# Attention of a fused kernel: value matmuls per head in one burst instead of one block per query tile, scores one tile ahead, partial blocks made full

## The chip, the cores and the metric

One core of one Trainium2 chip runs the whole program. The metric is the device time in microseconds of one execution. All data is float32; some matmul operands are rounded to a float32 form that TensorE takes in one pass (`F32R`), the others are streamed in two passes.

## The reference

Three stages in a row: attention with a threshold, a mixture of experts with one expert per token, and a second MLP. Only the first is touched by the change.

```python
def _attn_ref(q, k, v, tau):                 # q, k, v: (4, 8, 576, 64)
    scale = 1.0 / np.sqrt(q.shape[-1])
    scores = scale * np.matmul(q, k.transpose(0, 1, 3, 2))
    thresh = np.max(scores, axis=-1, keepdims=True) - tau
    scores = np.where(scores >= thresh, scores, -1000000000.0)
    scores = scores - np.max(scores, axis=-1, keepdims=True)
    attn = np.exp(scores)
    attn = attn / (np.sum(attn, axis=-1, keepdims=True) + 1e-09)
    return np.matmul(attn, v)
...
    x = attn_out.transpose(0, 2, 1, 3).reshape(B * S, H * D)
    x = _moe_ref(x=x, ...)                   # softmax gate, argmax expert, relu MLP
    return _moe2_ref(x=x, ...)               # g = h * sigmoid(1.702 h), second matmul
```

## The kernel before

Attention runs over 32 heads (4 sequences by 8 heads), taken in pairs; `b` is 0 or 1 within a pair. The 576 query rows of a head make five tiles of 128 rows, of which the last has 64 (`TPB` = 5, `LAST` = 64). A tile is a unit `n` of 160. Each engine has its own program, a Python loop written out for ten units of a pair and repeated over the pairs (`over_pairs`), and engines wait for each other on semaphores. There is no scheduler: the order on an engine is that of the code. Each engine works on a unit at another delay.

- POOL (`split_step`, lines 521 to 530) splits q and k into a rounded part and the rest, `qk_parts`, for a head two later. It also computes `thresh` (L568) and copies `vv` (L577, L578).
- TensorE, step of unit `n`: scores of `n` (L1140, four passes of 288 columns into one of two buffers `s_ps`); then `transpose`, which turns the probabilities of unit `n - 3` (four blocks at L1103, then three blocks of `qk_parts` at L1118, then the fifth block of probabilities at L1103) into `pt_ps`, which has one buffer; then the value block `j` of a unit eight back (L1167): two matmuls, of 256 and 320 columns, with 64 columns of `vv` as weights, one into the lower and one into the upper half of the partitions of `o_ps`. Five such blocks add up to a head.
- ScalarE: `copy_turned` copies `pt_ps` out (L939, L942 into `pT`, L947 into `qkT`), then the exponential of unit `n` (L968). In tile 2 of a head it also copies `o_ps` of an earlier head to `oT` (L962, L963).
- DVE: scores out of `s_ps` with their maximum (L662), the bias for the exponential (L666), then the mask of unit `n - 2` (L646), which multiplies the probabilities and sums them. In tile 4 it also writes x and the gate shares of an earlier head from `misc` ("x parts", L679 and L683), in tile 2 the sums' inverse (L692, L695).
- The turn (L1150) on TensorE, in tile 4: `oT` with an identity and the gate weights, three blocks of 128, 128 and 64 rows into `misc`.

What the others wait for: the transposes of unit `n - 3` wait for its mask (`probs_ready`) and for ScalarE's copy of the last ones (`keys_copied`, `turned_copied`); scores of `n` wait for the maximum of `n - 2` (`max_ready`). The semaphore `pv_block` counts value blocks.

Of the kernel before, what the change touches and what calls it, by code (L numbers as in the profile page):

```python
# [16 lines left out]
P = 128  # L17


def attention_moe_mlp_kernel(nc, q, k, v, tau, modality_id, w_gate, modality_bias, w1, w2, w_in, w_out, out):  # L20
# [45 lines left out]
    with ctx:  # L66
# [42 lines left out]
        placed[0] = max(placed[0], routing_end)  # L109
        oT = put("oT", [P, UP])  # L110

# [145 lines left out]
        pv_ready = sem("pv_ready")  # L257
        pv_block = sem("pv_block")
        oT_copied = sem("oT_copied")
# [110 lines left out]
        def _(sp):  # L370
# [63 lines left out]

            sp.wait_ge(pv_block, UNITS)
            sp.wait_ge(y_filled, (SLOTS - NT - 1) * 16)
# [73 lines left out]
        def _(pool):  # L510
# [49 lines left out]
            def step(pair):  # L560
                for b in range(2):
                    for t in range(TPB):
# [9 lines left out]
                        if t == 4:  # L572
                            head = pair * 2 + b
                            wait(pool, v_loaded[b], (pair + 1) * V_LOADS)

                            wait_apart(pool, pv_block, (head - 1) * TPB)
                            pool.tensor_copy(vv[b][:, 0:TPB - 1], v_in[b][:, 0:TPB - 1]).then_inc(v_copied, 1)  # L577
                            pool.tensor_copy(vv[b][0:LAST, TPB - 1], v_in[b][0:LAST, TPB - 1]).then_inc(v_copied, 1)  # L578
# [37 lines left out]
        def _(dve):  # L616
            dve.memset(row_sum[:], 1.0).then_inc(tau_ready, 1)
            for b in range(2):
                dve.memset(qk[b][LAST:P, TPB - 1], 0.0).then_inc(pads_cleared, 1)
                dve.memset(vv[b][LAST:P, TPB - 1], 0.0).then_inc(pads_cleared, 1)  # L620
            dve.memset(oT[0:DH, LOW:UP], 0.0).then_inc(pads_cleared, 1)
# [28 lines left out]
            def step(pair):  # L650
                for b in range(2):
                    for t in range(TPB):
# [3 lines left out]
                        if on(n, 0, UNITS):  # L656
# [268 lines left out]
        def _(act):  # L925
# [3 lines left out]

            def copy_turned(m, u, b, t, with_probs, with_qk):  # L930

                ub, ut = u // TPB, u % TPB
                w = rows(ut)
                if with_probs:
                    if ut == 0:

                        wait(act, pv_block, m - BEHIND - TPB)
                    act.wait_ge(keys_turned, m - BEHIND + 1)
                    act.copy(pT[ub][:, 0:TPB - 1, ut * P:ut * P + w], pt_ps[:, 0:TPB - 1, 0:w]).then_inc(keys_copied, 1)  # L939
# [10 lines left out]
            def step(pair):  # L950
                for b in range(2):
                    for t in range(TPB):
# [3 lines left out]
                        if on(n, 0, UNITS + 3):  # L956
                            copy_turned(n + AHEAD, (b * TPB + t - 3) % (2 * TPB), (b * TPB + t + AHEAD) // TPB % 2, (t + AHEAD) % TPB,
                                        on(n, 3, UNITS + 3), on(n, 0, UNITS - AHEAD))
# [12 lines left out]
            for m in range(AHEAD):  # L971
                copy_turned(m, 0, m // TPB, m % TPB, False, True)
            act.wait_ge(tau_ready, 5)
# [120 lines left out]
        def _(pe):  # L1094
            pe.wait_ge(consts, 3)

            def transpose(m, u, b, t, with_probs, with_qk):
# [25 lines left out]
            for m in range(AHEAD):  # L1123
                transpose(m, 0, m // TPB, m % TPB, False, True)

            def step(pair):
                for b in range(2):
                    for t in range(TPB):
                        n = pair * (2 * TPB) + b * TPB + t
                        head = pair * 2 + b  # L1130
                        r = rows(t)
                        if on(n, 0, UNITS):
                            if t == 0:

                                wait(pe, turned_copied, n + TPB)

                            wait(pe, max_ready, n - 1)
                            for c in range(2):
                                for part in (1, 2):
                                    mm = pe.matmul(s_ps[(b * TPB + t) % 2][:, c, 0:HALF], qkT[b][:, 0, t * P:(t + 1) * P],  # L1140
                                                   qkT[b][:, part, c * HALF:(c + 1) * HALF],
                                                   start=(part == 1), stop=(part == 2))
                            mm.then_inc(scores_ready, 1)
                        if t == 4 and on(head, 2, NH + 2):
                            wait(pe, oT_copied, head - 1)
                            wait(pe, x_written, (head - 2) * 4)
                            of_head = bass.ds((pair - 1) % (HEADS // 2) * 2 + b, 1)
                            for i in range(3):
                                w = min(P, UP - i * P)
                                mm = pe.matmul(misc[0:w, i * 2 * XW:(i + 1) * 2 * XW], oT[:, i * P:i * P + w],  # L1150
                                               turn_and_gate[:, of_head].rearrange("p a h w -> p (a h w)"),
                                               start=True, stop=True)
                            mm.then_inc(o_written, 1)
                        if on(n, 0, UNITS + 3):
                            transpose(n + AHEAD, (b * TPB + t - 3) % (2 * TPB), (b * TPB + t + AHEAD) // TPB % 2, (t + AHEAD) % TPB,
                                      on(n, 3, UNITS + 3), on(n, 0, UNITS - AHEAD))
                        if on(n, 8, UNITS + 8):
                            u = (b * TPB + t - 8) % (2 * TPB)
                            ub, j = u // TPB, u % TPB
                            if j == 0:  # L1160

                                wait(pe, keys_copied, n - 8 + TPB)
                                wait(pe, turned_copied, n - 8 + BEHIND + TPB)
                                wait(pe, v_copied, head * 2)
                                wait(pe, oT_copied, head - 1)
                            for lo, at, w in ((0, 0, LOW), (DH, LOW, UP)):
                                mm = pe.matmul(o_ps[lo:lo + DH, 0:w], vv[ub][:, j, :], pT[ub][:, j, at:at + w],  # L1167
                                               start=(j == 0), stop=(j == TPB - 1))
                            mm.then_inc(pv_block, 1)

            pe.wait_ge(pads_cleared, 7)
            pe.wait_ge(gate_loaded, 2 * 16)
            over_pairs(pe, step, PAIRS + 1)


# [153 lines left out]
```

## Time and profile before

| What | Value |
|---|---|
| Median of 3 runs | 1176.48 us (1175.52 to 1178.59) |
| Profiled execution | its span is 1178.2 us; no other time of it is given |
| TensorE busy, whole span | 1078.6 us, 92% |
| TensorE, DVE, ScalarE busy, 24 to 439 us | 405.09, 343.97, 323.96 of 415 us |
| Granted TensorE clock, 24 to 439 us | 1.00 (2.4 GHz) |
| First scores matmul, last x part of attention | 19.09 us, 438.95 us |
| Share of `DVE row_sum_eps L692` in the chain that ended last | 2% |

The span is the time from the first to the last instruction of the profiled execution, here 1.7 us above the median. TensorE's matmuls overlap each other in the records, so one row of several passes lasts longer than the distance to the next row; distances between starts tell what a piece takes. Attention fills the first 439 us of the span. Its ten-unit body repeats without change, so one pair of heads tells the rest.

### The profile page before, as it was taken

The page shows a single profiled execution, that of the slowest core. Times are in us where ns is not written, and L with a number is a line of the kernel's source. Part 1 is how long each engine was busy: PE and PEld are TensorE (multiplying, and loading weights), DVE is VectorE, ACT ScalarE, POOL GpSimd, SP SyncE. Part 2 cuts the span into 40 slices and gives each one's busy share as a digit, 9 for nine tenths or more (in the row PEclk, how much of TensorE's full clock was granted, in tenths as well). Part 3 has the DMA queues.
Part 4 walks back from the last instruction along what each step waited for, and adds up shares of the span by engine and source line. Part 5 has one row for each costly group of instructions (what it writes and reads, how often), then busy time and mean ns, then how long its engine had stood idle before and what let it go on. Part 6 is the DMA issues. An engine that isn't in the chain of part 4 may idle for free.

```text
span 1178.2 us, 19745 instructions
## 1 busy us (share of the span) xinstructions
PE 1078.6 (92%) x6008; PEld 862.0 (73%) x6009; DVE 575.5 (49%) x1421; ACT 522.0 (44%) x1086; POOL 251.3 (21%) x433
## 2 busy tenths in 40 slices
PE   4999999999999982779999969499999999999998
PEld 3666666666666642658888847389899999999997
DVE  3888888888888865411222232265322322222221
ACT  3887778777878750412222232254222222222222
POOL 5554455455445300000010100201001010100000
PEclk9999999999999995889999989699999999999999
DMA  3142211211122012991111114222001000000000
GB/s 68 40 155 50 55 40 42 48 45 40 45 50 50 21 31 79 244 28 43 45 45 45 36 50 155 89 82 63 27 2 53 0 27 27 27 27 0 27 1 27
DMA packets 99482, 59.68 MB, mean 51 GB/s; under 512 B 73984, under 2 KB 83200, under 8 KB 99456
## 3 DMA queue, kind: packets, MB, share of 16 engines
q1 hardware_dynamic: 93536, 44.15, 14.9%
q0 software_dynamic: 3040, 9.96, 3.2%
q10 hardware_dynamic: 2880, 5.24, 2.0%
q8 instruction: 14, 0.23, 0.1%
q14 instruction: 12, 0.10, 0.0%
HBM read 40.96 MB, written 18.37 MB: 50 GB/s over the span
## 4 chain that ended last, share of the span: by engine, by line
PE 79%; DVE 9%; issue 5%; DMA 3%; ACT 2%; DVEq 1%; POOL 1%; ACTq 0%; SPq 0%; POOLq 0%
PE s_ps L1283 17%; PE s_ps L1266 11%; PE s_ps L1200 9%; PE o_ps L1219 9%; PE s_ps L1140 7%; PE o_ps L1167 7%; PE pt_ps L1103 6%; PE o_ps L1266 6%; PE pt_ps L1118 4%; DVE scores L662 3%; DMA slot_x<-x_dram,slot_index 2%; DVE row_sum_eps L692 2%; PE misc L1150 1%; PE s_ps L1208 1%; DVE probs L646 1%
## 5 line engine op out<-in xcount | busy, mean ns | idle before, releaser
L906 DVE TENSOR_TENSOR g<-s_ps,sig 128x384 f32<-128x384 f32 x96 | 53.5, 558 | 276.2 <-ACT sig L1072 276.2
L1072 ACT ACTIVATE sig<-s_ps 128x384 f32<-128x384 f32 x96 | 47.2, 492 | 284.1 <-PE s_ps L1283 284.1
L662 DVE TENSOR_SCALAR_CACHE_REDUCE scores<-s_ps 128x576 f32<-128x576 f32 (+1 forms) x160 | 120.6, 754 | 66.5 <-PE s_ps L1140 41.0
L1140 PEld LDWEIGHTS s_ps<-qkT 128*128 128x128 f32 x640 | 91.4, 191 | 74.3 <-issue 64.9
L1103 PE MATMUL pt_ps<-ident,probs 128*128 128x128 f32 (+1 forms) x800 | 137.2, 271 | 7.3 <-DVE probs L646 7.3
L968 ACT ACTIVATE probs<-scores,neg_max,taus 128x576 f32<-128x576 f32 (+1 forms) x160 | 140.5, 878 | 2.9 <-DVE neg_max L666 0.8
L1283 PE MATMUL s_ps<-yT_high,w_in_high 128*128 (+1 forms) x384 | 131.9, 344 | 1.4 <-DVE yT_low L880 1.2
L1283 PE MATMUL s_ps<-yT_high,w_in_low 128*128 (+1 forms) x384 | 130.1, 339 | 0.0
L646 DVE SCALAR_TENSOR_TENSOR probs<-scores,thresh,probs 128x576 f32<-128x576 f32 (+1 forms) x160 | 129.9, 813 | 0.0
L1283 PE MATMUL s_ps<-yT_low,w_in_high 128*128 (+1 forms) x384 | 129.4, 337 | 0.0
L1140 PE MATMUL s_ps<-qkT 128*128 128x288 f32 x640 | 129.3, 325 | 0.0
L1167 PE MATMUL o_ps<-pT,vv 128*64 128x256 f32 (+1 forms) x640 | 120.8, 431 | 1.0 <-ACT oT L963 1.0
L939 ACT COPY pT<-pt_ps 128x512 f32<-128x512 f32 (+1 forms) x160 | 87.0, 544 | 68.4 <-PE pt_ps L1103 67.5
L1103 PEld LDWEIGHTS pt_ps<-ident,probs 128*128 128x128 f32 (+1 forms) x800 | 90.0, 140 | 31.5 <-DVE probs L646 15.7
L1118 PE MATMUL pt_ps<-ident,qk_parts 128*128 128x128 f32 x480 | 83.6, 285 | 14.1 <-POOL qk_parts L530 9.3
L947 ACT CAST qkT<-pt_ps 128x384 fp32r<-128x384 f32 x160 | 79.1, 494 | 6.8 <-PE pt_ps L1118 6.8
L821 DVE TENSOR_TENSOR slot_hT_low<-s_ps,slot_hT_high 128x512 fp32r<-128x512 f32 x38 | 24.5, 686 | 116.0 <-ACT slot_hT_high L988 116.0
L1200 PE MATMUL s_ps<-w_high,slot_xT_high 128*128 128x512 f32 x152 | 63.0, 414 | 17.0 <-DVE w_low L834 17.0
L1283 PEld LDWEIGHTS s_ps<-yT_high,w_in_high 128*128 128x128 f32 x384 | 72.7, 189 | 5.4 <-DVE yT_low L880 1.6
L1266 PE MATMUL s_ps<-w_out_high,g_low 128*128 128x512 f32 x192 | 76.2, 397 | 0.0
L1266 PE MATMUL s_ps<-w_out_low,g_high 128*128 128x512 f32 x192 | 75.8, 395 | 0.0
L568 POOL TENSOR_TENSOR thresh<-row_max,taus 128x1 f32<-128x1 f32 (+1 forms) x160 | 31.3, 196 | 206.8 <-DVE scores L662 206.6
(169 smaller groups left out, 1983.6 us busy)
## 6 DMA issues: line engine op xcount, KB each, us to landing
w_raw<-in_moe_w_dram SPq DMA_DIRECT2D x16, 512.0 KB, 4.7
y_dram<-slot_y ACTq DMA_DIRECT2D x19, 256.0 KB, 2.0
out_dram<-out_sb SPq DMA_DIRECT2D x6, 768.0 KB, 3.5
qk<-in_q_dram SPq DMA_DIRECT2D x32, 128.0 KB, 2.2
qk<-in_k_dram SPq DMA_DIRECT2D x32, 128.0 KB, 2.3
v_in<-in_v_dram SPq DMA_DIRECT2D x32, 128.0 KB, 2.2
x_dram<-x SPq DMA_DIRECT2D x16, 256.0 KB, 2.3
w_in_raw<-in_moe_w_in_dram SPq DMA_DIRECT2D x4, 1024.0 KB, 5.0
```

What stands on the lines that cost most here:

```text
L646: dve.scalar_tensor_tensor(out=probs[0:r, t, 0:SEQ], in0=scores[0:r, t], scalar=thresh[0:r, b, t:t + 1], in1=probs[0:r, t, 0:SEQ], op0=ALU ...
L662: dve.tensor_scalar(scores[0:r, t].rearrange("p (c n) -> p c n", c=2), s_ps[(b * TPB + t) % 2][0:r, :, 0:HALF], 1.0, None, ALU.mult, ALU.m ...
L939: act.copy(pT[ub][:, 0:TPB - 1, ut * P:ut * P + w], pt_ps[:, 0:TPB - 1, 0:w]).then_inc(keys_copied, 1)
L968: act.activation(probs[0:r, t, 0:SEQ], scores[0:r, t], ACT.Exp, bias=neg_max[0:r, b, t:t + 1], scale=taus[0:r, 2:3]).then_inc(exp_ready, 1)
L1103: return pe.transpose(pt_ps[:, j, 0:w], probs[0:w, ut, j * P:(j + 1) * P], ident[0:w, 0:w])
L1118: mm = pe.transpose(pt_ps[:, QK_AT + i], qk_parts[b][:, t, i].bitcast(F32), ident[:])
L1140: mm = pe.matmul(s_ps[(b * TPB + t) % 2][:, c, 0:HALF], qkT[b][:, 0, t * P:(t + 1) * P], qkT[b][:, part, c * HALF:(c + 1) * HALF], start=( ...
L1167: mm = pe.matmul(o_ps[lo:lo + DH, 0:w], vv[ub][:, j, :], pT[ub][:, j, at:at + w], start=(j == 0), stop=(j == TPB - 1))
L1200: mm = pe.matmul(slot_h_ps[:, c], x_part[:, a, :], w_part[:, a, cols], start=(a == 0 and part == 0), stop=(a == DB - 1 and part == 2))
L1219: mm = pe.matmul(o_ps[:], h_part[:, f, :], w_part[:, f], start=(f == 0 and part == 0), stop=(f == FB1 - 1 and part == 2))
L1266: mm = pe.matmul(mlp_y_ps[i], g_part[:, f % GT, at], w_part[:, f, :], start=(f == 0 and part == 0), stop=(f == FB2 - 1 and part == 2))
L1283: mm = pe.matmul(mlp_h_ps[f % 2], w_part[:, a, f * P:(f + 1) * P], y_part[:, bass.ds(c % 2 * DB + a, 1)].rearrange("p a b -> p (a b)"), st ...
```

## The change

The value matmuls leave the step of each unit. All five blocks of a head (ten matmuls) now stand in one burst, `values_of`, in tile 3 of the next head, behind that step's scores. The scores of a unit are issued one step earlier in the code (`scores_of(n + 1)` behind the transposes of step `n`), which is the same order as before among scores and transposes. The copy of `o_ps` on ScalarE moves from tile 2 to tile 4, the turn on TensorE from tile 4 to tile 0, the x parts on DVE from tile 4 to tile 2 (in front of the mask of tile 0). The transposes of the last, 64-row tile and the third block of the turn become full 128 by 128 blocks; their unused rows are cleared once at the start.

```diff
+            dve.memset(oT[:], 0.0).then_inc(pads_cleared, 1)
+            dve.memset(probs[LAST:P, TPB - 1, 0:SEQ], 0.0).then_inc(pads_cleared, 1)
...
-                        if t == 4 and on(head, 2, NH + 2):
+                        if t == 2 and on(head, 2, NH + 2):
                             wait(dve, o_written, head - 1)
...
-                        if t == 2 and on(head, 2, NH + 2):
-                            wait(act, pv_block, (head - 1) * TPB)
-                            wait(act, o_written, head - 2)
+                        if t == 4 and on(head, 1, NH + 1):
+                            wait(act, pv_heads, head)
+                            wait(act, o_written, head - 1)
                             act.copy(oT[0:DH, 0:LOW], o_ps[0:DH, 0:LOW])
...
-                    return pe.transpose(pt_ps[:, j, 0:w], probs[0:w, ut, j * P:(j + 1) * P], ident[0:w, 0:w])
+                    return pe.transpose(pt_ps[:, j, :], probs[:, ut, j * P:(j + 1) * P], ident[:])
...
+            def values_of(head, b):
+
+                wait(pe, keys_copied, (head + 1) * TPB)
+                wait(pe, turned_copied, head * TPB + BEHIND + TPB)
+                wait(pe, v_copied, (head + 1) * 2)
+                wait(pe, oT_copied, head)
+                for j in range(TPB):
+                    for lo, at, w in ((0, 0, LOW), (DH, LOW, UP)):
+                        mm = pe.matmul(o_ps[lo:lo + DH, 0:w], vv[b][:, j, :], pT[b][:, j, at:at + w],
+                                       start=(j == 0), stop=(j == TPB - 1))
+                mm.then_inc(pv_heads, 1)
...
-                        if on(n, 8, UNITS + 8):
-                            u = (b * TPB + t - 8) % (2 * TPB)
-                            ub, j = u // TPB, u % TPB
...
+                        if on(n, 0, UNITS - 1):
+                            scores_of(n + 1, (b * TPB + t + 1) // TPB % 2, (t + 1) % TPB)
+                        if t == 3 and on(head, 1, NH + 1):
+                            values_of(head - 1, 1 - b)
+                        if t == 0 and on(head, 2, NH + 2):
+                            turn_rows(head - 2, bass.ds((pair - 1) % (HEADS // 2) * 2 + b, 1))
```

TensorE before, in the loop over pairs, first head, from the transposes of tile 3's step to those of tile 4's: `pt_ps` are transposes, `o_ps` value blocks, `s_ps` scores, `misc` the turn.

```order
L1103 MATMUL pt_ps<-ident,probs 128x128
L336 ISA [waits turned_copied,keys_copied]
L336 REGISTER_ALU [waits v_copied]
L1167 MATMUL o_ps<-pT_55,vv_61 64x256 [waits oT_copied]
L1167 MATMUL o_ps<-pT_55,vv_61 64x320
L336 REGISTER_ALU
L1140 MATMUL s_ps<-qkT_51 128x288 [waits max_ready]
L1140 MATMUL s_ps<-qkT_51 128x288 x3
```

TensorE after, same place in the program.

```order
L1134 MATMUL s_ps<-qkT_51 128x288 [waits max_ready]
L1134 MATMUL s_ps<-qkT_51 128x288 x3
L336 REGISTER_ALU
L336 ISA [waits keys_copied]
L336 REGISTER_ALU [waits turned_copied]
L1147 MATMUL o_ps<-pT_55,vv_61 64x256 [waits oT_copied,v_copied]
L1147 MATMUL o_ps<-pT_55,vv_61 64x320
...
L1103 MATMUL pt_ps<-ident,probs 128x128 [waits keys_copied,probs_ready]
L1103 MATMUL pt_ps<-ident,probs 128x128 x3
```

Where one block stood between the transposes of tile 0 and the scores of tile 4, ten matmuls (the pair of `o_ps` rows five times) now stand behind those scores and in front of the transposes of tile 1.

DVE before, second head of a pair, tile 2 and the masks around it.

```order
L662 TENSOR_SCALAR scores,row_max<-s_ps 128x576 [waits thresh_ready,probs_ready,exp_ready,scores_ready]
L666 TENSOR_SCALAR neg_max<-row_max,taus 128x1 [waits max_ready]
L646 SCALAR_TENSOR_TENSOR probs,row_sum<-scores,thresh,probs 128x576 [waits thresh_ready,exp_ready]
L336 ISA
L692 TENSOR_SCALAR row_sum_eps<-row_sum 128x5 [waits probs_ready]
L695 RECIPROCAL row_inv<-row_sum_eps 128x5 [waits sum_eps]
```

DVE after, same tile.

```order
L663 TENSOR_SCALAR scores,row_max<-s_ps 128x576 [waits thresh_ready,probs_ready,exp_ready,scores_ready]
L667 TENSOR_SCALAR neg_max<-row_max,taus 128x1 [waits max_ready]
L680 ISA [waits inv_ready,o_written]
L680 TENSOR_TENSOR x<-misc,row_inv 128x4x64
L684 ISA
L684 TENSOR_SCALAR x<-misc,row_inv 64x64
L680 ISA
L680 TENSOR_TENSOR shares<-misc,row_inv 128x4x8
L684 ISA
L684 TENSOR_SCALAR shares<-misc,row_inv 64x8
L647 SCALAR_TENSOR_TENSOR probs,row_sum<-scores,thresh,probs 128x576 [waits thresh_ready,exp_ready]
L336 ISA
```

The four instructions of the x parts now stand between the bias of tile 2 and the mask of tile 0; the two of the inverse stay behind that mask.

## Rows read from the trace of the kernel before

**Rows 1.** DVE's groups, one long stretch (150 to 410 us): busy us, mean ns, idle before.

```profile
L692 DVE TENSOR_SCALAR row_sum_eps<-row_sum 128x5 f32<-128x5 f32 x20 | 30.4, 1518 | 0.0
```

**Rows 2.** TensorE's timeline, 212 to 220 us: start us, us, engine, line, operation.

```profile
213.56 0.80 PE L1140 MATMUL s_ps<-qkT 128*128 128x288 f32 x4
...
216.05 0.81 PE L1140 MATMUL s_ps<-qkT 128*128 128x288 f32 x4
...
217.45 0.27 PE L1103 MATMUL pt_ps<-ident,probs 128*128 128x128 f32 x1
217.66 0.76 PE L1167 MATMUL o_ps<-pT,vv 128*64 128x256 f32 x4
218.34 0.80 PE L1140 MATMUL s_ps<-qkT 128*128 128x288 f32 x4
```

**Rows 3.** The chain that ended last, 214.5 to 229.1 us: the turn.

```profile
219.15 0.88 PE misc L1150 x6
```

**Rows 4.** Timeline where scores lead to DVE's L662: start of program, and loop.

```profile
29.86 0.49 PE L1118 MATMUL pt_ps<-ident,qk_parts 128*128 128x128 f32 x3
...
31.03 0.76 DVE L662 TENSOR_SCALAR_CACHE_REDUCE scores<-s_ps 128x576 f32<-128x576 f32 x1
...
200.34 0.80 PE L1140 MATMUL s_ps<-qkT 128*128 128x288 f32 x4
...
201.38 0.76 DVE L662 TENSOR_SCALAR_CACHE_REDUCE scores<-s_ps 128x576 f32<-128x576 f32 x1 [0.51 <-ACT probs L968]
```

**Rows 5.** Timeline of the stage's end: single value block, then four in a row.

```profile
430.75 0.76 PE L1167 MATMUL o_ps<-pT,vv 128*64 128x256 f32 x4
...
431.55 0.37 ACT L962 COPY oT<-o_ps 64x256 f32<-64x256 f32 x1 [0.26 <-PE o_ps L1167]
...
433.88 0.48 PE L1167 MATMUL o_ps<-pT,vv 128*64 128x320 f32 x1
...
436.28 0.37 ACT L962 COPY oT<-o_ps 64x256 f32<-64x256 f32 x1 [3.94 <-PE o_ps L1167]
```

**Rows 6.** Timeline: POOL's splitting (L530) and DVE beside it, at three places.

```profile
7.59 1.53 POOL L530 TENSOR_TENSOR qk_parts<-qk,qk_parts 128x640 fp32r<-128x640 f32 x1
...
24.62 2.17 POOL L530 TENSOR_TENSOR qk_parts<-qk,qk_parts 128x640 fp32r<-128x640 f32 x1
...
26.23 1.18 DVE L646 SCALAR_TENSOR_TENSOR probs<-scores,thresh,probs 128x576 f32<-128x576 f32 x1
...
202.19 0.21 DVE L666 TENSOR_SCALAR neg_max<-row_max,taus 128x1 f32<-128x1 f32 x1
...
202.45 2.08 POOL L530 TENSOR_TENSOR qk_parts<-qk,qk_parts 128x640 fp32r<-128x640 f32 x1
```

**Rows 7.** Timeline: DVE's x parts in both heads of a pair, what follows them.

```profile
207.36 0.20 DVE L666 TENSOR_SCALAR neg_max<-row_max,taus 64x1 f32<-64x1 f32 x1
...
208.69 0.80 DVE L646 SCALAR_TENSOR_TENSOR probs<-scores,thresh,probs 128x576 f32<-128x576 f32 x1
...
209.55 0.66 PE L1103 MATMUL pt_ps<-ident,probs 128*128 128x128 f32 x4 [0.31 <-DVE probs L646]
...
210.25 0.59 ACT L939 COPY pT<-pt_ps 128x512 f32<-128x512 f32 x1 [0.93 <-PE pt_ps L1103]
...
220.36 0.21 DVE L666 TENSOR_SCALAR neg_max<-row_max,taus 64x1 f32<-64x1 f32 x1
...
221.41 0.80 DVE L646 SCALAR_TENSOR_TENSOR probs<-scores,thresh,probs 128x576 f32<-128x576 f32 x1
```

**Rows 8.** ScalarE's timeline, 215.4 to 218.6 us, with the copies of o_ps.

```profile
215.57 0.48 ACT L947 CAST qkT<-pt_ps 128x384 fp32r<-128x384 f32 x1
...
216.98 0.87 ACT L968 ACTIVATE probs<-scores,neg_max,taus 128x576 f32<-128x576 f32 x1
217.87 0.59 ACT L939 COPY pT<-pt_ps 128x512 f32<-128x512 f32 x1
...
218.51 0.50 ACT L947 CAST qkT<-pt_ps 128x384 fp32r<-128x384 f32 x1
```

More of the change, by code:

```diff
@@ L109, in attention_moe_mlp_kernel @@
         placed[0] = max(placed[0], routing_end)
-        oT = put("oT", [P, UP])
+        oT = put("oT", [P, 3 * P])
         turn_and_gate = put("turn_and_gate", [P, HEADS, 2, XW])
@@ L257, in attention_moe_mlp_kernel @@
         pv_ready = sem("pv_ready")
-        pv_block = sem("pv_block")
+        pv_heads = sem("pv_heads")
         oT_copied = sem("oT_copied")
@@ L432, in _ @@
             step(PAIRS)
-            sp.wait_ge(pv_block, UNITS)
+            sp.wait_ge(pv_heads, NH)
             sp.wait_ge(y_filled, (SLOTS - NT - 1) * 16)
@@ L574, in step @@
                             wait(pool, v_loaded[b], (pair + 1) * V_LOADS)
-                            wait_apart(pool, pv_block, (head - 1) * TPB)
+                            wait_apart(pool, pv_heads, head - 1)
                             pool.tensor_copy(vv[b][:, 0:TPB - 1], v_in[b][:, 0:TPB - 1]).then_inc(v_copied, 1)
@@ L928, in _, with copy_turned @@
             act.dma_start(y_dram[(SLOTS - 1) * P:SLOTS * P], zeros[:]).then_inc(slot_y_stored, 16)
-            def copy_turned(m, u, b, t, with_probs, with_qk):
+            def copy_turned(head, m, u, b, t, with_probs, with_qk):
                 ub, ut = u // TPB, u % TPB
@@ L935, in copy_turned @@
                     if ut == 0:
-                        wait(act, pv_block, m - BEHIND - TPB)
+                        wait(act, pv_heads, head - 1)
                     act.wait_ge(keys_turned, m - BEHIND + 1)
@@ L956, in step @@
                         if on(n, 0, UNITS + 3):
-                            copy_turned(n + AHEAD, (b * TPB + t - 3) % (2 * TPB), (b * TPB + t + AHEAD) // TPB % 2, (t + AHEAD) % TPB,
+                            copy_turned(head, n + AHEAD, (b * TPB + t - 3) % (2 * TPB), (b * TPB + t + AHEAD) // TPB % 2, (t + AHEAD) % TPB,
                                         on(n, 3, UNITS + 3), on(n, 0, UNITS - AHEAD))
-                        if t == 2 and on(head, 2, NH + 2):
-                            wait(act, pv_block, (head - 1) * TPB)
-                            wait(act, o_written, head - 2)
+                        if t == 4 and on(head, 1, NH + 1):
+                            wait(act, pv_heads, head)
+                            wait(act, o_written, head - 1)
                             act.copy(oT[0:DH, 0:LOW], o_ps[0:DH, 0:LOW])
@@ L1124, in _, with scores_of, turn_rows @@
                 transpose(m, 0, m // TPB, m % TPB, False, True)
+            def scores_of(n, b, t):
+                if t == 0:
+                    wait(pe, turned_copied, n + TPB)
+                wait(pe, max_ready, n - 1)
+                for c in range(2):
+                    for part in (1, 2):
+                        mm = pe.matmul(s_ps[(b * TPB + t) % 2][:, c, 0:HALF], qkT[b][:, 0, t * P:(t + 1) * P],
+                                       qkT[b][:, part, c * HALF:(c + 1) * HALF],
+                                       start=(part == 1), stop=(part == 2))
+                mm.then_inc(scores_ready, 1)
+            def values_of(head, b):
[8 more added lines that the diff above has]
+                mm.then_inc(pv_heads, 1)
+            def turn_rows(head, of_head):
+                wait(pe, oT_copied, head + 1)
+                wait(pe, x_written, head * 4)
+                for i in range(3):
+                    mm = pe.matmul(misc[:, i * 2 * XW:(i + 1) * 2 * XW], oT[:, i * P:(i + 1) * P],
+                                   turn_and_gate[:, of_head].rearrange("p a h w -> p (a h w)"),
+                                   start=True, stop=True)
+                mm.then_inc(o_written, 1)
             def step(pair):
@@ L1130, in step @@
                         head = pair * 2 + b
[L1131 to L1153, printed above, removed]
                         if on(n, 0, UNITS + 3):
@@ L1156, in step @@
                                       on(n, 3, UNITS + 3), on(n, 0, UNITS - AHEAD))
-                        if on(n, 8, UNITS + 8):
-                            u = (b * TPB + t - 8) % (2 * TPB)
-                            ub, j = u // TPB, u % TPB
[L1160 to L1171, printed above, removed]
+                        if on(n, 0, UNITS - 1):
[4 more added lines that the diff above has]
+                            turn_rows(head - 2, bass.ds((pair - 1) % (HEADS // 2) * 2 + b, 1))
+            pe.wait_ge(pads_cleared, 8)
             pe.wait_ge(gate_loaded, 2 * 16)
+            scores_of(0, 0, 0)
             over_pairs(pe, step, PAIRS + 1)
```

3 lines of the change are left out of this document (1 added, 2 removed).

## The prediction

> **What bounds the kernel now.** I read first the grouped rows of a long stretch: one head's DVE instruction comes 20 times in 260 us, so a head takes 13.00 us [rows 1]; with 32 heads the attention stage is over a third of the time, and nothing behind it changes. Then I read TensorE's own timeline, because its busy share there is near full [rows 2]. A query tile with its scores, transposes and value block takes 2.29 us (216.05 to 218.34), of which the value block is 0.68 (217.66 to 218.34). A tile whose transposes are the partial ones takes 2.49 (213.56 to 216.05), and the turn 0.88 [rows 3]. A head is thus 4 x 2.29 + 2.49 + 0.88 = 12.53 us of TensorE, and the other 0.47 are waits on DVE's chain. So TensorE bounds the stage, with little to spare behind it: the question is which chain runs 13 us per head once TensorE's share shrinks.
>
> **The change, part by part.**
>
> *Value blocks in a burst.* Inside the loop a block stands between unlike matmuls. The last transpose before it is followed only 0.21 us later (217.45 to 217.66), where transposes follow each other at 0.11: three passes last 0.49 and one 0.27, so (0.49 - 0.27)/2 [rows 2, 4]. That is 0.10 for going over to 64-column blocks; I take as much for going back, in the first scores pass. The end of the program shows blocks back to back already [rows 5]: one block, from its start to ScalarE's copy of o_ps, is 0.80 (430.75 to 431.55); four are 2.40 (433.88 to 436.28), so each further block costs 0.53. A burst of five is then 0.68 + 4 x 0.53 = 2.80, and 2.90 with the way in, against 5 x 0.68 + 10 x 0.10 = 4.4 now. Bounds: 0.48 a block if only the streaming of 1152 columns counted at 2.4 GHz, 0.68 if nothing is gained: 2.7 to 3.5.
>
> *Full blocks.* The last tile's transposes save 2.49 - 2.29 = 0.20, the turn about as much (its narrow third block has the same two changes of shape). The two memsets lie on DVE at the start, ahead of POOL's splitting, which ends at 7.59 + 1.53 = 9.12 and which the first transposes wait for [rows 6]: nothing, at worst 1 us.
>
> TensorE's work per head becomes 5 x (1.61 - 0.20) for scores and transposes (216.05 to 217.66, less both changes of shape), + 2.90 + 0.68 = 10.6 us. If it stayed the bound, that would be a large gain.
>
> The Trainium skill, page TensorEngine Tiling (Array Packing), Tiling Modes, Key Properties, says that changing the tiling mode drains TensorE. The trace agrees in the 0.21 beside 0.11; that rule alone speaks for the change, and its result is the last rival below.
>
> *What the burst does to the others.* TensorE goes in order. The burst stands between the transposes of tile 0 and those of tile 1, which are what ScalarE works from; pt_ps has one buffer, so ScalarE cannot be ahead, and it runs dry. I follow the new order round once, from the burst of one head to the next, with durations that the trace shows; every link is a wait that the code has.
> 1. Burst, 2.90.
> 2. Transposes of tile 1 until ScalarE's L939: 209.55 to 210.25, 0.70 [rows 7].
> 3. ScalarE L939 to L947: 217.87 to 218.51, 0.64 [rows 8].
> 4. L947, then both oT copies (new place: tile 4), to the exponential: 215.57 to 216.98, 1.41 [rows 8].
> 5. Exponential to next L939: 216.98 to 217.87, 0.89 [rows 8].
> 6. Tile 2: L939 to L947 again 0.64; its cast 0.50 + 0.05 until TensorE may overwrite pt_ps: 1.19 together.
> 7. Second half of tile 3's transposes, then scores of the next head's tile 2, to DVE's L662: 29.86 to 31.03, 1.17, a place without value blocks [rows 4]; + 0.06 since they start from a wait (the four passes at 209.55, such a start, last 0.66: three gaps of (0.66 - 0.27)/3 = 0.13 instead of 0.11 [rows 2, 7]). In the first head of a pair DVE sets wait registers first: 200.34 to 201.38 is 1.04, 0.10 of it the slower first pass, so 0.94, against 1.17 - 4 x 0.11 = 0.73: 0.21 more there.
> 8. L662 to L666: 201.38 to 202.19, 0.81 [rows 4, 6].
> 9. x parts, now in front of the mask of tile 0: L666 to L646, 1.33 in the first head (207.36 to 208.69), 1.05 in the second (220.36 to 221.41) [rows 7].
> 10. L646 to the transposes it releases: 208.69 to 209.55, 0.86 [rows 7].
> 11. Those transposes and the scores behind them, up to the next burst: 1.61 - 0.20 + 0.06 = 1.47.
>
> Sum without 9: 2.90 + 0.70 + 0.64 + 1.41 + 0.89 + 1.19 + 1.23 + 0.81 + 0.86 + 1.47 = 12.10. Second head of a pair 13.15; first 12.10 + 1.33 + 0.21 = 13.64; mean 13.40.
>
> *POOL against the mask.* POOL L530 lasts 1.53 where DVE is idle and 2.08 or 2.17 where a mask L646 runs [rows 6]; a mask that starts inside it (26.23, POOL until 24.62 + 2.17 = 26.79) lasts 1.18, not 0.80, and ends 0.62 behind POOL's end. L692 lasts 1.52 in every head [rows 1]: it comes behind the mask, while L530 runs. So these share something, and whoever comes second waits. Today the mask starts just ahead of L530. Afterwards the x parts stand between L666 and the mask, and L530 goes first: it starts 0.26 behind L666 (202.19 to 202.45) and ends 1.79 behind; the mask ends 0.62 later, at 2.41, instead of 1.05 + 0.80 = 1.85 or 1.33 + 0.80 = 2.13. That adds 0.56 and 0.28, mean 0.42. L692's wait nearly vanishes, but DVE had room there.
> The Trainium skill, GPSIMD Engine Reference, Key points, says the same of the cause: GpSimd shares its SBUF interfaces with VectorE, in contention with DVE instructions of two SBUF inputs or in a 2-port mode. It gives no price; L646 has two such inputs, x's tensor_tensor one. It speaks against this change, and without it the period would be 13.40.
>
> *Sum.* 13.40 + 0.42 = 13.82 per head, + 0.82; 31 periods lie between the 32 bursts: + 25.4 us. At the end the last head no longer waits behind the copy and turn of the one before (431.55 to 433.88 [rows 5]): - 2.3. Together + 23. Against the profiled execution's span of 1178.2 this is 1201; the median of the runs is 1.7 lower: **1199 us**. TensorE would stand idle some 3 us per head, ScalarE about as long under the burst.
>
> **Rivals.**
> - *Chain, but the mask is not held up* (DVE gets in first, or the x parts fill less). For it: in the loop of before masks were never delayed. Against: the start order. 31 x 0.40 - 2.3 = + 10: 1187. Chance 0.20.
> - *DVE's leg is hidden, faster.* If the mask of tile 0 were ready before ScalarE is through tile 4's copies, the cycle would be ScalarE's: 2.90 + 0.70 + 0.64 + 1.41 + 0.89 = 6.54, two tiles at 0.64 + 0.50 + 0.89 = 2.03 at most, 0.42 for the copy of tile 4, 1.47: 12.5. 31 x -0.5 - 2.3 = - 18: 1159. It decides from 0.9 us less on DVE's leg than I count; ten links argue against. Chance 0.08.
> - *The burst streams no better than blocks apart* (0.68 each): 0.6 more per head, + 42: 1218. Against it stands the end of the program. Chance 0.07.
> - *Both sides cancel*, period 12.95 to 13.2 after the end's gain: 1173 to 1180. Needs most links a little short. Chance 0.06.
> - *TensorE stays the bound*, gains by the removed changes of shape alone: 10.6 per head, 31 x -2.4 - 2.3: about 1100. It needs pt_ps's single buffer and DVE's chain never to be waited for. Chance 0.03.
> - The forecast itself: 0.56.
>
> **Numbers.** About 0.3% (3.5 us) is what a measurement of this kernel tells from none. Slower: 0.56 + 0.20 + 0.07 = 0.83; same 0.06; faster 0.11. Range: down to the rival without the hold-up and its own spread (0.1 per head), up to the forecast with every link 0.03 long: 1184 to 1209, which leaves out some 2 in 10.
>
> **What would show it.** Period of L693 13.8 (two values in turn, near 13.7 and 13.9). o_ps passes of a burst 2.8 us from first start to the next transposes. ScalarE's largest idle time in front of L939, ended by the transposes of tile 1, over 2 us once a head. L647 behind the x parts 1.1 to 1.35 long, L693 short. TensorE waiting in front of tile 0's transposes for probs L647. If the waits before the transposes are all ended by ScalarE, the DVE leg was wrong; if the mask is 0.81 everywhere, the hold-up was.

## The result, and the profile after

The changed kernel takes 1196.34 us (median of 4 runs, 1193.66 to 1201.27), the kernel before 1177.53 us in the same comparison: ratio 1.018, 95% interval 1.0155 to 1.0206. Slower by 19 us; the interval lies wholly above 1. Its profiled execution has a span of 1193.4 us and a time of 1195.5 us.

First the answer to [rows 1] and to the table of before: DVE's group in 150 to 410 us (busy us, mean ns, idle before), the waits of 100 to 400 us (us in total, times, longest), and the busy us of PE, PEld, DVE, ACT and POOL in that stretch, first of the kernel before, then of the changed one.

```profile
L693 DVE TENSOR_SCALAR row_sum_eps<-row_sum 128x5 f32<-128x5 f32 x19 | 3.0, 159 | 0.0
```

```profile
ACT pT L939 <- PE pt_ps L1103: 83.2, 44, 2.4
DVE scores L663 <- PE s_ps L1134: 65.1, 45, 2.5
PEld pt_ps L1103 <- DVE probs L647: 47.2, 33, 2.0
```

```profile
100.00:400.00 300.00, 296.26 (x1986) 201.30 (x1985) 252.13 (x716) 237.54 (x508) 150.96 (x254) 1.00 0.19 44
```

```profile
100.00:400.00 300.00, 252.74 (x1896) 210.31 (x1895) 223.37 (x685) 215.41 (x485) 140.52 (x242) 1.00 0.18 43
```

19 heads instead of 20 fit into 260 us. TensorE is busy 252.74 of 300 us, where it was 296.26: it has become the engine that waits for VectorE, while ScalarE waits up to 2.4 us and VectorE up to 2.5 us for TensorE. Three engines wait for each other in turn, at full clock (1.00, which is 2.4 GHz). L693 is no longer held: 159 ns, where it was 1518.

Now one head in the timeline of after, from burst to burst; it answers to [rows 7, 8] and holds every link of the predicted chain.

```profile
199.40 2.91 PE L1147 MATMUL o_ps<-pT,vv 128*64 128x256 f32 x20
...
202.24 0.66 PE L1103 MATMUL pt_ps<-ident,probs 128*128 128x128 f32 x4
...
202.94 0.59 ACT L939 COPY pT<-pt_ps 128x512 f32<-128x512 f32 x1 [2.44 <-PE pt_ps L1103]
...
203.58 0.50 ACT L947 CAST qkT<-pt_ps 128x384 fp32r<-128x384 f32 x1
...
203.95 0.38 ACT L962 COPY oT<-o_ps 64x256 f32<-64x256 f32 x1
...
204.78 0.87 ACT L968 ACTIVATE probs<-scores,neg_max,taus 64x576 f32<-64x576 f32 x1
...
205.68 0.59 ACT L939 COPY pT<-pt_ps 128x512 f32<-128x512 f32 x1
...
206.87 0.54 PE L1118 MATMUL pt_ps<-ident,qk_parts 128*128 128x128 f32 x3
...
208.30 0.76 DVE L663 TENSOR_SCALAR_CACHE_REDUCE scores<-s_ps 128x576 f32<-128x576 f32 x1 [0.50 <-PE s_ps L1134]
...
209.10 0.21 DVE L667 TENSOR_SCALAR neg_max<-row_max,taus 128x1 f32<-128x1 f32 x1
...
210.45 1.07 DVE L647 SCALAR_TENSOR_TENSOR probs<-scores,thresh,probs 128x576 f32<-128x576 f32 x1
...
211.59 0.66 PE L1103 MATMUL pt_ps<-ident,probs 128*128 128x128 f32 x4 [1.75 <-DVE probs L647]
...
213.15 2.35 PEld L1147 LDWEIGHTS o_ps<-pT,vv 128*64 128x64 f32 x20 [0.17 <-issue]
```

Burst to burst is 13.75 us (199.40 to 213.15) here and 13.52 in the next head (to 226.67). The largest idle times of ScalarE and of TensorE are the two that the prediction named: ScalarE 2.44 before L939, TensorE 1.75 before tile 0's transposes. The last rows show GpSimd beside the mask, in the first head of a pair (its mask is the row at 210.45 above) and in the second.

```profile
209.37 1.54 POOL L530 TENSOR_TENSOR qk_parts<-qk,qk_parts 128x640 fp32r<-128x640 f32 x1
...
222.63 0.21 DVE L667 TENSOR_SCALAR neg_max<-row_max,taus 128x1 f32<-128x1 f32 x1
...
222.89 1.55 POOL L530 TENSOR_TENSOR qk_parts<-qk,qk_parts 128x640 fp32r<-128x640 f32 x1
...
223.68 1.38 DVE L647 SCALAR_TENSOR_TENSOR probs<-scores,thresh,probs 128x576 f32<-128x576 f32 x1
```

L530 starts 0.27 and 0.26 behind L667, now before the mask, and lasts 1.54 and 1.55, near its undisturbed 1.53, where it was 2.08 [rows 6]. The mask ends at 211.52 and 225.06, 0.61 and 0.62 behind the end of L530: it is the one that waits now.

### The profile page after: what moved, and what is told of

The parts are those of the page before. It is cut to its first block, busy times and chain, and to the rows that moved or that the text cites. A ratio compares the mean times of both kernels' runs of the same rounds, so it can differ in the third digit from the quotient of the medians.

```text
span 1193.4 us, 19773 instructions
## 1 busy us (share of the span) xinstructions
PE 1037.5 (87%) x6008; PEld 888.5 (74%) x6009; DVE 554.5 (46%) x1422; ACT 507.1 (42%) x1086; POOL 247.9 (21%) x433
## 4 chain that ended last, share of the span: by engine, by line
PE 73%; DVE 10%; issue 6%; ACT 5%; DMA 3%; DVEq 1%; ACTq 1%; POOL 1%; SPq 0%; POOLq 0%
PE s_ps L1289 17%; PE s_ps L1272 11%; PE o_ps L1225 8%; PE s_ps L1206 8%; PE o_ps L1147 8%; PE pt_ps L1103 6%; PE o_ps L1272 6%; PE s_ps L1134 4%; DVE probs L647 3%; DVE scores L663 3%; PE pt_ps L1118 3%; DMA y_dram<-slot_y 2%; ACT pT L939 2%; PE s_ps L1214 1%; DVEq L680 1%
## 5 line engine op out<-in xcount | busy, mean ns | idle before, releaser
L1103 PE MATMUL pt_ps<-ident,probs 128*128 128x128 f32 x800 | 143.7, 279 | 67.2 <-DVE probs L647 50.0
L663 DVE TENSOR_SCALAR_CACHE_REDUCE scores<-s_ps 128x576 f32<-128x576 f32 (+1 forms) x160 | 120.7, 754 | 104.4 <-PE s_ps L1134 101.2
L1103 PEld LDWEIGHTS pt_ps<-ident,probs 128*128 128x128 f32 x800 | 90.4, 140 | 103.4 <-DVE probs L647 67.8
L647 DVE SCALAR_TENSOR_TENSOR probs<-scores,thresh,probs 128x576 f32<-128x576 f32 (+1 forms) x160 | 147.5, 922 | 2.5 <-ACT probs L968 2.5
L968 ACT ACTIVATE probs<-scores,neg_max,taus 128x576 f32<-128x576 f32 (+1 forms) x160 | 143.6, 898 | 1.9 <-DVE neg_max L667 1.1
L939 ACT COPY pT<-pt_ps 128x512 f32<-128x512 f32 (+1 forms) x160 | 88.3, 552 | 117.0 <-PE pt_ps L1103 116.0
L1134 PE MATMUL s_ps<-qkT 128*128 128x288 f32 x640 | 125.1, 317 | 0.0
L1147 PE MATMUL o_ps<-pT,vv 128*64 128x320 f32 (+1 forms) x640 | 93.2, 411 | 0.5 <-ACT pT L939 0.5
L568 POOL TENSOR_TENSOR thresh<-row_max,taus 128x1 f32<-128x1 f32 (+1 forms) x160 | 45.6, 285 | 228.7 <-DVE scores L663 228.6
L947 ACT CAST qkT<-pt_ps 128x384 fp32r<-128x384 f32 x160 | 81.4, 509 | 6.5 <-PE pt_ps L1118 6.5
L1147 PEld LDWEIGHTS o_ps<-pT,vv 128*64 128x64 f32 x640 | 60.8, 136 | 20.3 <-issue 4.9
```

The source lines that it names most:

```text
L647: dve.scalar_tensor_tensor(out=probs[0:r, t, 0:SEQ], in0=scores[0:r, t], scalar=thresh[0:r, b, t:t + 1], in1=probs[0:r, t, 0:SEQ], op0=ALU ...
L663: dve.tensor_scalar(scores[0:r, t].rearrange("p (c n) -> p c n", c=2), s_ps[(b * TPB + t) % 2][0:r, :, 0:HALF], 1.0, None, ALU.mult, ALU.m ...
L968: act.activation(probs[0:r, t, 0:SEQ], scores[0:r, t], ACT.Exp, bias=neg_max[0:r, b, t:t + 1], scale=taus[0:r, 2:3]).then_inc(exp_ready, 1)
L1103: return pe.transpose(pt_ps[:, j, :], probs[:, ut, j * P:(j + 1) * P], ident[:])
L1147: mm = pe.matmul(o_ps[lo:lo + DH, 0:w], vv[b][:, j, :], pT[b][:, j, at:at + w], start=(j == 0), stop=(j == TPB - 1))
```

## The experiments

All numbers of the runs stand in one table, because whole-program times blur them. Period: the start of a head's row_inv on VectorE and the start of the same instruction 16 heads later, divided by 16. Stage end: start of the last x part. From there to the end of the span, where no experiment changes a line, the profiled executions take between 731.4 us (full blocks alone) and 739.9 (x parts behind the mask), so up to 8 us between two of those executions are not the edit's, and the period and the stage's end tell more than the median. Each ratio is to the kernel before as it ran in the same comparison (medians 1177.11 to 1178.4).

| Kernel | row_inv starts, 16 heads apart | Period | Stage end | Median | Ratio to before (95%) |
|---|---|---|---|---|---|
| before | 152.60, 360.60 | 13.00 | 438.95 | 1177.53 | |
| after | 143.39, 361.50 | 13.63 | 456.75 | 1196.34 | 1.018 (1.0155 to 1.0206) |
| e1: x parts behind mask | 145.11, 339.43 | 12.15 | 413.64 | 1153.85 | 0.9788 (0.9757 to 0.9818) |
| e2: L530 in tile 1 | 141.56, 352.93 | 13.21 | 448.21 | 1187.7 | 1.0074 (1.0044 to 1.0105) |
| e3: before + full blocks | 152.27, 360.27 | 13.00 | 438.46 | 1177.87 | 0.9999 (0.9973 to 1.0024) |
| e4: after, partial blocks | 142.68, 360.98 | 13.64 | 456.13 | 1197.68 | 1.0173 (1.0137 to 1.021) |
| e5: before, L530 in tile 1 | 151.05, 357.46 | 12.90 | 436.29 | 1176.88 | 0.9989 (0.9967 to 1.001) |
| e6: e5 + full blocks | 149.81, 353.28 | 12.72 | 431.19 | 1169.01 | 0.9929 (0.9912 to 0.9945) |
| e7: e1, burst 3 + 2 | 141.37, 330.35 | 11.81 | 401.86 | 1143.31 | 0.9722 (0.9697 to 0.9746) |
| e8: burst 2 + 2 + 1, x in tile 4 | 144.92, 339.10 | 12.14 | 411.52 | 1149.67 | 0.9768 (0.9746 to 0.979) |
| e9: before, inverse in tile 3 | 149.93, 353.34 | 12.71 | 429.42 | 1167.62 | 0.9919 (0.9886 to 0.9951) |
| e10: e9 + full blocks | 147.11, 344.96 | 12.37 | 419.81 | 1160.73 | 0.9868 (0.9828 to 0.9909) |
| e11: e7, inverse in tile 3 | 142.73, 331.63 | 11.81 | 402.01 | 1141.87 | 0.9689 (0.9648 to 0.973) |
| e12: e8, inverse in tile 3 | 140.80, 328.38 | 11.72 | 398.48 | 1139.67 | 0.9685 (0.9647 to 0.9724) |

**e1, the x parts.** Link 9 and the hold-up are put off the chain by one move.

```diff
+                        if on(n, 2, UNITS + 2):
+                            last = (b * TPB + t - 2) % (2 * TPB)
+                            mask(pair if b * TPB + t >= 2 else pair - 1, last // TPB, last % TPB)
                         if t == 2 and on(head, 2, NH + 2):
                             wait(dve, o_written, head - 1)
...
-                        if on(n, 2, UNITS + 2):
-                            last = (b * TPB + t - 2) % (2 * TPB)
-                            mask(pair if b * TPB + t >= 2 else pair - 1, last // TPB, last % TPB)
```

> The changed kernel, with the four x parts on VectorE behind the mask of tile 0 instead of in front of it; nothing else. Theory (the chain of eleven links with VectorE's leg sets the period, and link 9 and the hold-up of the mask by GpSimd are on it): x parts (1.35 and 1.05) and hold-up (0.27 and 0.57) leave the chain, 1.62 less per head; but ScalarE's own cycle (rival of the prediction, 12.5) takes over first, so the period falls from 13.64 to about 12.4: 31 x -1.2 = -37, about 1159 us, mask of tile 0 at 0.80. Rival A (the burst itself starves the other engines and the place of the x parts does not matter): no change, 1196. Rival B (TensorE's work is what counts, 10.6 per head): no change either. If the x parts are on the chain but there is no lower floor: 13.64 - 1.62 = 12.0, about 1146.

```profile
203.31 0.21 DVE L667 TENSOR_SCALAR neg_max<-row_max,taus 128x1 f32<-128x1 f32 x1
...
203.44 0.81 DVE L647 SCALAR_TENSOR_TENSOR probs<-scores,thresh,probs 128x576 f32<-128x576 f32 x1
...
203.58 2.09 POOL L530 TENSOR_TENSOR qk_parts<-qk,qk_parts 128x640 fp32r<-128x640 f32 x1
...
216.58 0.66 PE L1103 MATMUL pt_ps<-ident,probs 128*128 128x128 f32 x4 [0.28 <-DVE probs L647]
```

In the timeline of e1 the mask starts 0.13 behind L667 and ahead of L530, lasts 0.81, and L530 is the one that is stretched. The period falls by 1.49 and the kernel is 2.1% faster than before. So four small instructions in front of one mask, with the hold-up that they bring about, cost the change 42 us: rivals A and B fall.

The expected floor of 12.4 was not met either. 1.49 is all that there was to win: the 1.62 counted from L667 to the mask (1.35 and 1.05), and 0.13 of that way is still there. The transposes of tile 0 still wait for VectorE's mask, as the row at 216.58 shows, and e1's chain of waits (200 to 226 us) goes from L663 over L667 and the mask to these transposes in both heads:

```profile
204.18 0.10 DVE probs L647
204.27 0.04 issue
204.31 0.66 PE pt_ps L1103 x4
...
216.44 0.10 DVE probs L647
216.53 0.04 issue
216.58 0.66 PE pt_ps L1103 x4
```

So the chain of e1 is that of the changed kernel without link 9 and the hold-up. ScalarE's own cycle was not reached.

**e2, GpSimd's L530 out of the mask's way.**

```diff
-                elif t == 2:
+                if t == 1:
                     wait(pool, parts_ready, head * PARTS + 3)
                     pool.tensor_tensor(both[:, :, 2], twice, both[:, :, 1].bitcast(F32), ALU.subtract
```

> The changed kernel, with GpSimd's last splitting step (L530) issued one tile earlier, in tile 1, right behind the other of that tile, so that it has ended when the mask of tile 0 runs behind the x parts. Theory (the mask of tile 0 waits for GpSimd's instruction): this mask goes back from 1.07 and 1.38 to 0.80, the period falls by 0.27 and 0.57, mean 0.42: 31 x -0.42 = -13, about 1183 us. Rival (the mask's length is no wait for GpSimd, or something else lets the transposes go): 1196. A delay of thresh in tile 1 behind the longer row of GpSimd would take some of the gain.

The period falls by 0.42, the predicted amount. The stage ends only 8.5 us sooner, not 13: heads at either end have no such mask to win back, and at the start two masks are now hit that were not (the second at 33.70 us). Of the missing 4.5 us, 1.7 lie behind the last row_inv; why is open. Timeline of e2, start of the program:

```profile
23.47 1.53 POOL L530 TENSOR_TENSOR qk_parts<-qk,qk_parts 128x640 fp32r<-128x640 f32 x1
23.55 2.07 DVE L647 SCALAR_TENSOR_TENSOR probs<-scores,thresh,probs 128x576 f32<-128x576 f32 x1
```

The mask starts 0.08 late and pays 1.27 for it; it ends (25.62) 0.62 behind L530 (25.00). The cause of the hold-up is shown by both runs: it goes with the order of two starts.

**e3 and e4, the full blocks alone and taken back.**

```diff
-                    return pe.transpose(pt_ps[:, j, 0:w], probs[0:w, ut, j * P:(j + 1) * P], ident[0:w, 0:w])
+                    return pe.transpose(pt_ps[:, j, :], probs[:, ut, j * P:(j + 1) * P], ident[:])
...
-                                w = min(P, UP - i * P)
-                                mm = pe.matmul(misc[0:w, i * 2 * XW:(i + 1) * 2 * XW], oT[:, i * P:i * P + w],
+                                mm = pe.matmul(misc[:, i * 2 * XW:(i + 1) * 2 * XW], oT[:, i * P:(i + 1) * P],
```

> The kernel before, with only the partial blocks of the last tile's transposes and of the turn made full (and the two memsets that this needs). Theory (TensorE bounds the kernel before; a partial tile takes 0.20 more than a full one and the turn about 0.2 more): 0.40 less per head, 32 x -0.40 = -13, about 1165 us; the period falls from 13.00 to 12.6. Rival (VectorE's chain stands right behind TensorE, as the 0.47 of waits per head suggest): half of it or less, 1171 to 1177.

> The changed kernel with the partial blocks kept as they were before (transposes of the 64-row tile and the third block of the turn), the burst and all else as changed. Theory (TensorE has some 3 us per head of idle time, and neither the transposes of tile 4 nor the turn is one of the eleven links): within 0.3% of the changed kernel, 1196. Rival (TensorE's work still counts): 0.40 more per head, 1209.

e4 came as expected. e3 did not: the period stays at 13.00 to the hundredth, so TensorE's work alone did not bound the kernel before. Its chain of waits, start and us of each piece, says what did:

```profile
201.07 0.78 DVE scores L663 x2
...
202.82 1.43 DVE row_sum_eps L693
...
204.58 0.78 DVE scores L663 x2
```

The chain passes through row_sum_eps, held for 1.43 us (by L530, as e5 shows below). Two tiny instructions, the inverse of the sums, keep VectorE from the next scores. The chain of the kernel before has the same piece (200 to 227 us), but in the first head of each pair only, where e3 has it in every head; the prediction read that chain only from 214.5 us on, and passed over the 2% that the table of before gives for it:

```profile
203.13 1.44 DVE row_sum_eps L692
```

**e5 and e6: L530 moved in the kernel before** (the edit of e2), without and with the full blocks.

> The kernel before, with GpSimd's last splitting step (L530) one tile earlier, in tile 1; all else as before. The run with full blocks alone left the period at 13.00, and its chain of waits passes through row_sum_eps, held for 1.43 us once a head. New theory (before, VectorE's chain with that hold-up set the period, TensorE stood just behind it, with 12.53 by the sum of the prediction): row_sum_eps goes from 1.52 to some 0.15, the period falls to TensorE's, about 12.5 to 12.6: 31 x -0.45 = -14, about 1163 us. Theory of the prediction (TensorE bounds the kernel before, VectorE has room there): 13.00 and no change, 1177.

> The kernel before with both: GpSimd's last splitting step in tile 1, and the blocks made full. New theory: with the hold-up gone TensorE is the bound, and then the full blocks count: 0.40 per head less than with the step moved alone, period about 12.1 to 12.3, 1150 to 1157 us, although the full blocks alone gave nothing. Rival (the 0.40 is no time of TensorE's, the full block costs what the partial one did): as with the step moved alone. Had TensorE bound the kernel before, the two together would give just what the full blocks gave alone, which is nothing.

Neither number came. In the DVE groups (150 to 410 us) the reason stands, the masks of the kernel before first, then two groups of e5:

```profile
L646 DVE SCALAR_TENSOR_TENSOR probs<-scores,thresh,probs 128x576 f32<-128x576 f32 (+1 forms) x100 | 80.7, 807 | 0.0
```

```profile
L646 DVE SCALAR_TENSOR_TENSOR probs<-scores,thresh,probs 128x576 f32<-128x576 f32 (+1 forms) x102 | 92.8, 909 | 0.0
...
L692 DVE TENSOR_SCALAR row_sum_eps<-row_sum 128x5 f32<-128x5 f32 x21 | 3.3, 159 | 0.0
```

row_sum_eps is free, but the masks have grown from 807 ns to 909 in the mean, 0.5 us per head: the hold-up was moved, not removed. e5 is inconclusive on the bound; the next pair leaves L530 where it is and moves what it hits.

**e9 and e10: the inverse moved in the kernel before**, behind the mask of tile 3's step, when L530 has ended; without and with the full blocks.

```diff
-                        if t == 2 and on(head, 1, NH + 1):
+                        if t == 3 and on(head, 1, NH + 1):
 
                             wait(dve, probs_ready, head * TPB)
                             dve.tensor_scalar(row_sum_eps[:, 1 - b], row_sum[:, 1 - b], 1e-9, None,
```

> The kernel before, with the sum's inverse on VectorE (L692 and L695, row_sum_eps and row_inv) behind the mask of tile 3's step instead of tile 2's; GpSimd's splitting untouched, and at that time done. Theory (before, TensorE was busy 12.78 of the 13.00, and VectorE's chain through row_sum_eps, held 1.43 us by GpSimd's L530, made the other 0.22; the earlier run that moved L530 only moved the hold-up onto another mask): row_sum_eps falls from 1.52 to about 0.16 with no mask getting longer, period 12.8 in both heads of a pair, 31 x -0.2 = -6, about 1171 us. Theory of the prediction (VectorE has room there): 13.00, no change.

> The kernel before, with the inverse in tile 3 and the blocks made full. Theory: VectorE's chain is then out of the way and TensorE alone sets the period, so that the full blocks count for the first time: 12.78 - 0.3 to 0.4 = 12.4 to 12.5, 31 x -0.55 = -17, about 1160 us. Rival (another chain through VectorE's masks or ScalarE's copies ends at 12.7, where the run with both L530 moved and full blocks stood): 12.7, 1168.

In the chain of waits of e9 (200 to 228 us) there is only one engine:

```profile
by line: PE s_ps L1140 28.7%; PE o_ps L1167 25.6%; PE pt_ps L1103 23.2%; PE pt_ps L1118 13.6%; PE misc L1150 9.4%
...
200.97 0.88 PE misc L1150 x6
201.85 0.59 PE pt_ps L1103 x4
...
202.87 0.69 PE o_ps L1167 x4
203.56 0.73 PE s_ps L1140 x4
204.29 0.44 PE pt_ps L1103 x4
...
213.66 0.88 PE misc L1150 x6
```

From turn to turn TensorE takes 12.69 us without a gap, and 12.74 in the next head (213.66 to 226.40). That is its true work per head in the kernel before, 12.71 in the mean, and 0.3 of the 13.00 was VectorE held by GpSimd. With that gone the full blocks count, 12.71 to 12.37, where in e3 they counted nothing. In e10 TensorE is not alone any more: its chain goes through VectorE's scores, inverse and x parts once in each pair (219.42 to 224.51 us), now with row_sum_eps at 0.09.

**e7 and e8: a shorter burst.** e7 is e1 with three blocks in tile 3 and two in tile 4; e8 has two, two and one, and the x parts in tile 4.

```diff
                         if t == 3 and on(head, 1, NH + 1):
-                            values_of(head - 1, 1 - b)
-                        if t == 0 and on(head, 2, NH + 2):
+                            values_of(head - 1, 1 - b, 0, 3)
+                        if t == 4 and on(head, 1, NH + 1):
+                            values_of(head - 1, 1 - b, 3, 5)
+                        if t == 1 and on(head, 2, NH + 2):
                             turn_rows(head - 2, bass.ds((pair - 1) % (HEADS // 2) * 2 + b, 1))
```

> The changed kernel with the x parts behind the mask (as in the first run), and the burst cut in two: three value blocks in tile 3, two in tile 4; the copy of o_ps moves to tile 0 of the next head and the turn to tile 1. Theory (a burst of 2.84 starves ScalarE and VectorE, shorter bursts less): the period falls from 12.14 by 0.1 to 0.3, some -3 to -9 us, 1145 to 1151, and no idle time of ScalarE in front of L939 is longer than 1.5 us. Rival (the length of the burst does not matter, only where the copies and x parts stand): 12.14 or a little more by the added change of shape, 0.2 a head, 1154 to 1160.

> The changed kernel with the x parts back in tile 4, and the burst cut in three: two blocks in tile 3, two in tile 4, one in tile 0 of the next head; copy of o_ps in tile 1, turn in tile 2. Theory (as above): 0.2 to 0.4 less than 12.14 per head, 1142 to 1148 us. Rival: three changes to 64-column blocks and back cost 0.4 more of TensorE per head than one, and since TensorE is then busy 11.0 of 12.1 nothing is left to gain: 1154 or more.

ScalarE's waits for the transposes, in e1 and then in e7 (100 to 400 us):

```profile
ACT pT L939 <- PE pt_ps L1103: 37.6, 26, 2.2
```

```profile
ACT pT L939 <- PE pt_ps L1103: 45.1, 52, 1.1
```

Twice as many waits and none over 1.1 us, though more in total, and 0.34 less per head, slightly more than expected. TensorE's share of the chain of waits (200 to 226 us) rises from 59% in e1 to 78% in e7: with shorter waits of the others in between, its own work comes nearer to being the bound. That speaks for the length of the burst; the copy and the turn had to move with it, and no run tells their share. e8 stayed at 12.14, above its range; its chain of waits had this piece in one head of a pair:

```profile
216.24 1.44 DVE row_sum_eps L693
```

**e11 and e12: e7 and e8 with the inverse in tile 3.**

> The kernel with the burst cut 3 + 2 and the x parts behind the mask, and the inverse in tile 3. There row_sum_eps was held 0.68 in the mean, and no piece of the chain of waits was on it. Theory: period stays at 11.8 (12.07 and 11.56), within 2 us of 1143. Rival (any hold-up of VectorE counts): 0.5 less per head, 1128.

> The kernel with the burst cut 2 + 2 + 1 and the x parts in tile 4, and the inverse in tile 3. There row_sum_eps was held 1.33 and lay on the chain (1.44 us of one head of a pair). Theory: with the hold-up gone the period falls from 12.14 to what ScalarE's copies and TensorE allow, 11.7 to 11.9, 1136 to 1143 us. Rival (the added changes of shape set it): 12.1, 1149.

Both as the theory had it. TensorE's share of the chain of e12 (200 to 226 us) is 87%. Where row_sum_eps was off the chain, moving it gave nothing (11.81 and 11.81); where it was on it, 0.42 per head. e11 and e12 are the fastest, 3.1% under the kernel before; their intervals overlap, so which of them is better stays open.

## Why the prediction was right, and where it was off

Slower, by 19 us where 23 were forecast, and 1196.3 against 1199: the chain of the prediction was the chain. That the absolute time is only 3 us off is in small part luck: the kernel before was 1 us slower in this comparison than in the runs the forecast starts from. Its links in the head shown above, which is the first of a pair:

| Link | Predicted | Measured |
|---|---|---|
| 1 burst | 2.90 | 2.84 |
| 2 transposes to L939 | 0.70 | 0.70 |
| 3 L939 to L947 | 0.64 | 0.64 |
| 4 L947, copies, to exponential | 1.41 | 1.20 |
| 5 to next L939 | 0.89 | 0.90 |
| 6 to TensorE may go on | 1.19 | 1.19 |
| 7 second half, scores, to L663 | 1.44 | 1.43 |
| 8 L663 to L667 | 0.81 | 0.80 |
| 9 x parts | 1.33 | 1.35 |
| 10 mask to transposes | 0.86 + 0.28 | 1.14 |
| 11 to the next burst | 1.47 | 1.56 |
| Sum | 13.92 | 13.75 |

**The sum of the links.** Three terms were mis-sized. Link 4 is 0.21 shorter: in the kernel before 0.58 passed between the start of L947 and the first copy (215.57 [rows 8] to the row below), here 0.37 (203.58 to 203.95); the new place of the copies is cheaper, and I had carried the old place's time along. The burst is 0.06 shorter. Link 11 is 0.09 longer: 0.17 of idle time stands in front of the burst, ended by "issue" (instructions for registers and waits), which I had left out. In the second head 13.52 against 13.71. Mean 0.18 less than predicted, 31 times: 5.6 us.

```profile
216.15 0.37 ACT L962 COPY oT<-o_ps 64x256 f32<-64x256 f32 x1
```

**The end of the stage.** It is 17.8 us later than before (456.75 and 438.95); 31 periods longer by 0.63 make 19.5, so start and end gave back 1.7, where I had 2.3.

**The mask's hold-up** was right in place, order and size (0.27 and 0.57 to 0.58 over 0.80; e2 took 0.42 off the period). The Trainium skill, page SBUF — State Buffer, section Who interferes with whom, states the rule behind it: VectorE and GpSimd share a port pair under an exclusive lock, and whoever issues first keeps it for the whole instruction. The traces agree: the mask ahead by 0.14 (e1) runs undisturbed and L530 lasts 2.09; L530 ahead by 0.08 (e2) lasts 1.53 and the mask 2.07.

**The burst.** The saving was real, and the chains give it in full: one block 0.69 (e9), five 2.84. What follows a block is dearer too, scores 0.73 (e9) against 0.53, transposes 0.59 against 0.44. Five apart are 5 x (0.69 + 0.20) = 4.45, one burst 2.84 + 0.15 = 2.99; I had 4.4 and 2.90. The chain of e7, with its records of a burst partly missing:

```profile
212.78 1.76 PE o_ps L1147 x11
214.55 0.59 PE pt_ps L1103 x4
...
215.57 0.53 PE s_ps L1134 x4
216.11 1.23 PE o_ps L1147 x8
```

Three blocks 1.76, two 1.23: each further block 0.53 to 0.54, as [rows 5] had it.

**"So TensorE bounds the stage" was wrong**, although it did no harm to the forecast, which went by the other chain. The sum of 12.53 per head was too small too: e9 gives 12.69 and 12.74, mainly because the transposes behind the turn are among those that last 0.59. And "L692's wait nearly vanishes, but DVE had room there" was wrong for the kernel before: that wait, 1.5 us a head, lay on its chain in one head of each pair, and e9 gains 0.8% by moving two instructions away from it. It is right for the kernel after, whose chain goes elsewhere.

**Full blocks** were put into TensorE's share and at nothing on the chain, and e4 shows nothing. On TensorE they are worth 0.49 per head, where 0.40 was estimated: 0.19 in the transposes of the last tile (1.07 in e9, 208.87 to 209.94, against 0.88 of full ones), 0.15 in the turn and 0.15 behind it. The period of e10 gives 0.34 of it, since its chain goes through VectorE in part.

**The rivals.** The one called hidden leg, with ScalarE's cycle of 12.5 as the bound, is out, and its sum was too long: e1 runs at 12.15 with VectorE's leg, shorter by 1.49, still the one that TensorE waits for. Of the excess, at least 0.35, link 4 and the burst explain 0.27; where the rest lies no run shows. The prediction held that 0.9 less on VectorE's leg would decide for ScalarE, and 1.49 did not. The others are out too: the mask was held up, the burst streams at 0.53, TensorE stands idle 47 of 300 us.

## What to carry to other kernels

Gathering matmuls into one burst saves time of TensorE, which shortens the kernel only where TensorE bounds. Here the engines that live from its small outputs ran dry meanwhile (ScalarE for up to 2.4 us at a time), and the bursts cut in two or three (e11, e12) gave the shortest periods. When a small instruction is moved on VectorE, look at what it now stands in front of, and at which of VectorE's and GpSimd's long instructions then starts first. Before calling an engine the bound by its busy share, follow the chain of waits through a whole period, and look for a tiny instruction with a long duration: it is a wait that no wait row shows.

## What was not expected of the hardware

- A VectorE instruction on 128x5 elements with one input from SBUF (row_sum_eps) is held until GpSimd's instruction ends, 1.52 us instead of 0.16. The Trainium skill, page SBUF — State Buffer, section Who interferes with whom, counts tensor_scalar among the operations that can contend with GpSimd, when their operands meet conditions; the traces show the wait and do not tell the mode.
- A mask that is held ends 0.61 to 0.62 behind GpSimd's end at every place (after, and e2), though it lasts 0.80 alone: part of its duration passes while it waits.
- A turn whose last block has 64 columns of weights makes the transposes behind it 0.59 long (e9), against 0.44 behind a full one. The chain of waits of e10:

```profile
209.22 0.73 PE misc L1150 x6
209.95 0.44 PE pt_ps L1104 x4
```

  The full block is worth 0.15 in the turn itself (0.88 to 0.73) and 0.15 behind it. The Trainium skill, TensorEngine Tiling (Array Packing), Key Properties, says that a change of mode drains TensorE; these prices would fit that, but no run here separates a drain from another cause.
